# Attention and two expert layers on one core: layer two's first expert taken from a row's choice, gate columns spread during routing, expert lists on VectorE

## The chip, the cores and the metric

The kernel runs on one core of a Trainium2 chip. The metric is the device time of one execution in microseconds (us), the median of several runs. Engines are called TensorE (PE in the profile; PEld is its weight load), VectorE (DVE), ScalarE (ACT), GpSimd (POOL) and SyncE (SP, which here only issues DMAs).

## The reference, cut to what matters

```python
# attention: 4 batches, 8 heads, 768 rows, head width 64; 8 global keys and a band of 96
x = attention(q, k, v)                    # 3072 rows x 512
def layer(x, w_gate, w1, w2, bias):       # 8 experts, w1 512x1024, w2 1024x512 each, float32
    logits = x @ w_gate + bias            # bias only in layer two, by each row's modality
    e = argmax(logits, axis=1)
    for expert in range(8):
        rows = (e == expert)
        if rows.any():
            out[rows] = gate[rows] * (relu(x[rows] @ w1[expert]) @ w2[expert])
```

Layer one, then layer two on its output. The counts of rows by expert follow from the inputs. When the reference is computed, layer one's experts 0 to 7 get 455, 416, 361, 397, 367, 410, 395 and 271 rows. Layer two's get 0, 1503, 0, 1556, 13, 0, 0 and 0. The first row that layer one sends to its expert 0 is row 1, and layer two sends that row to its expert 3.

## The kernel before, in words

**Stages.** Attention runs first (`banded_attention`, which is taken for these sizes; `general_attention` is code for other sizes that every engine jumps over). Then `routing(0)`, `mixture(0)`, `routing(1)` and `mixture(1)`.

**Routing.** `find_rows` on VectorE takes each row's best expert, counts the tiles of 128 rows that each expert needs (`t.te`), and gives each expert its first tile (`t.tb`). One-hot matrices `t.ob` and `t.val` are written; TensorE multiplies them (`count_and_rows`) into the table of source rows, from which the first gather index `t.gidx` comes. In layer two a line forces the count of expert 0 to at least one: `t.te[:, 0, 0:1]` is maximised with 1.0. Expert 0's weights are loaded before layer two's routing is known, and its first tile is always tile 0. `list_experts` on GpSimd makes the list of active experts (`t.e_i`), of their first tiles (`t.tb_i`) and their number (`t.na_i`). All engines wait for it (`s.listed`) before they enter the mixture. `sum_values` on TensorE turns gates and destinations into slots' order; in layer one it stands ahead of the first tile's matmuls, in layer two behind them.

**Mixture.** Tiles of 128 slots are worked on one after another. For tile i TensorE does `up(i)` (24 matmuls, L1080), `turn_x(i+1)` (transposes of the next tile's rows, L1069), `down(i-1)` (24 matmuls, L1100) and `turn_h(i)` (transposes of h, L1088). ScalarE makes h (L1176), the high part of x (L1162) and of h (L1182). VectorE makes the low parts (x: L1198, h: L1246) and the scaled result y (L1226), and in layer one it weighs y with the gate columns `t.wg2` of layer two (L1218), from which layer two's logits come.

**Weights.** An expert's weights are 8 chunks of 512 KB. SP loads them into four stage buffers. In the first tile of an expert, ScalarE copies the eight chunks of the *next* expert into the other half of `t.W` (L1170) and VectorE writes their low parts (L1207, `w_low`). Chunks 1 to 4 stand before the h work of that tile on both engines, chunks 5 to 8 behind it. Chunk 5's load waits until chunk 1's low part is written. In the last expert of layer one, the next expert is layer two's first one. Its first four chunks are issued as soon as the last expert's own weights are split, which is in an earlier expert's tiles.

**Gate columns.** `load_gate2` (SP, L928) broadcasts layer two's gate matrix over 128 partitions into `t.q` and `t.k` once attention is stored. `spread_gate2` (ScalarE, L938) reorders it into `t.wg2`. Since `t.wg2` shares memory with the one-hot tables, it waits for layer one's `sum_values` (`tabled` 2), and stands between the first `x_high` and the first tile's h on ScalarE.

**Attention's end.** `add_logits(B - 1, NPR - 1)` adds the last pair's share of layer one's logits on VectorE (L460). Then VectorE leaves the block, loads the flag `t.banded`, and jumps over the code of `general_attention` to `find_rows` (L758).

Of the kernel before, what the change touches and what calls it, by code (L numbers as in the profile page):

```python
# [30 lines left out]
LISTS = 7  # L31
# [46 lines left out]
def setup_block(nc, t, s, q, k, v, n_global, n_local, w_gate, w_gate2, mod_bias):  # L78

    with nc.Block() as block:  # L80
# [15 lines left out]
        def _(pool):  # L96
            pool.memset(t.ones[:, :], 1.0).then_inc(s.consts, 1)
            pool.memset(t.ident[:, :], 0.0).then_inc(s.consts, 1)
            pool.memset(t.v[:, :, :, DH:VW], 1.0).then_inc(s.consts, 1)
# [12 lines left out]
            pool.wait_ge(s.consts, 2)  # L112
# [44 lines left out]
def banded_attention(t, s, q, k, v, x1, x2, w1, w2, modality_id):  # L157
# [219 lines left out]
    def vector(dve):  # L377
        flag = dve.value_load(t.banded[0:1, 0:1], min_val=0, max_val=1)
        with dve.If_eq(dve.to_reg(flag), 1):
# [117 lines left out]
            add_logits(B - 1, NPR - 1)  # L497
            dve.wait_ge(s.logits_moved, NPR * B + 1)
# [48 lines left out]
    return gpsimd, sync, tensor, vector, scalar  # L547
# [178 lines left out]
def routing(t, s, layer):  # L726
# [6 lines left out]
    st = s.route[layer]  # L733
    L = t.logits[:, 0:nt, :] if layer == 0 else t.logits2[:, 2:2 + nt, :]
# [7 lines left out]
    group = lambda g: t.val[:, 0:nt, g, :]  # L742
    within, total = t.PS[:, 0, 0:nt * E], t.PS[:, 1, 1:1 + nt * E]
    before = t.PS[:, 1, 0:nt * E]

# [10 lines left out]
    def find_rows(dve):  # L756
# [42 lines left out]
        if layer:  # L799
            link(dve, dve.tensor_tensor(col(3), col(3), t.far[:, :], ALU.add))  # L800
# [3 lines left out]
        dve.wait_ge(st.slot_known, 1)  # L804
        place = t.iota_row[:, 0:E + 1].unsqueeze(2).to_broadcast([P, E + 1, E])
# [6 lines left out]
        for i0, i1 in pieces:  # L812
            dve.tensor_tensor(t.ob[:, i0:i1, :], t.iota_row[:, :].unsqueeze(1).to_broadcast([P, i1 - i0, P]),  # L813
                              t.c[:, 2, i0:i1].unsqueeze(2).to_broadcast([P, i1 - i0, P]), ALU.is_equal)\
               .then_inc(st.placed, 1)
# [46 lines left out]
    def list_experts(pool):  # L862
        count = [LISTS * layer]

        def then(ins):

            count[0] += 1
            ins.then_inc(s.listed, 1)
            pool.wait_ge(s.listed, count[0])

        order = t.act[:, 1, :]
        pool.wait_ge(st.ordered, 2)
        a = t.lists[:, :, :, :]
        then(pool.tensor_copy(t.na_i[:, layer:layer + 1], order[:, E:E + 1]))
        then(pool.tensor_tensor(a, a, t.te[:, :, :].unsqueeze(2).to_broadcast([P, 2, E + 1, E]), ALU.mult))

        for w in (4, 2, 1):
            then(pool.tensor_tensor(a[:, :, :, 0:w], a[:, :, :, 0:w], a[:, :, :, w:2 * w], ALU.add))  # L878
        then(pool.tensor_copy(t.tb_i[:, :], a[:, 0, :, 0:1].rearrange("p a e -> p (a e)")))
        then(pool.tensor_copy(t.e_i[:, :], a[:, 1, :, 0:1].rearrange("p a e -> p (a e)")))  # L880

    def exps_and_rows(act):
# [9 lines left out]
        act.activation(t.ob[:, 0:by_act, :], t.apart[:, 0:by_act, :], ACT.Relu, bias=t.ones_f[:, 0:1], scale=-1.0)\  # L892
           .then_inc(st.placed_act, 1)

    def count_and_rows(pe):
        pe.wait_ge(st.chosen, 1)
# [4 lines left out]
        for n, (i0, i1) in enumerate(pieces + [(0, by_act)]):  # L901
            if n < 2:
                pe.wait_ge(st.placed, 2 + n)
            else:
                pe.wait_ge(st.placed_act, 1)
            for i in range(i0, i1):
                last = pe.matmul(t.PS[:, 2, 0:2 * MAXT], t.ob[:, i, :], t.val[:, i, 0:2, :]
                                 .rearrange("p g a -> p (g a)"), start=i == pieces[0][0], stop=i == by_act - 1)
# [680 lines left out]
```

## Time and profile before

| | us |
|---|---|
| median of 3 runs | 1084.35 |
| lowest and highest | 1084.23 and 1086.38 |
| the profiled execution | 1084.99 |
| its span | 1083.3 |
| TensorE matmul busy in it | 977.4 |
| VectorE busy | 619.4 |
| ScalarE busy | 406.5 |
| GpSimd busy | 184.3 |

Start times in the rows below are microseconds from the span's start. A row of the timeline merges neighbours of one kind (x4 is four instructions). Its bracket says how long the engine had been idle before the row and what released it.

### The profile page before, as it was taken

To read this page: it belongs to the slowest core of one execution; us is meant where nothing else is said; L and a number is where in the kernel's file an instruction comes from. 1 tells how busy PE (TensorE), PEld (TensorE's weight loads), DVE (VectorE), ACT (ScalarE), POOL (GpSimd) and SP (SyncE) were. 2 spreads that over 40 slices of the span, in tenths; PEclk is the share of its full clock that TensorE was granted. 3 is DMA by queue.
4 is the path that set the end of the run, shared out by engine and by line. 5 is a ranking of instruction groups with operands and counts; after the bars stand their busy time and mean duration, and the time that the engine had idled before them with its cause. 6 is when DMAs were issued, how large, how long until landed. Compare 5 with 4: busy or idle time off the path is not lost.

```text
span 1083.3 us, 19099 instructions
## 1 busy us (share of the span) xinstructions
PE 977.4 (90%) x5416; PEld 828.4 (76%) x5417; DVE 619.4 (57%) x1584; ACT 406.5 (38%) x735; POOL 184.3 (17%) x275
## 2 busy tenths in 40 slices
PE   4999999999248999999999999356999999999995
PEld 3999999998246888888888888245888888888884
DVE  6666666665439697896987969837322225222221
ACT  3655555553244333343352533206322225222220
POOL 1291000000041111111111111032212112121111
PEclk9999999999569999999999999768999999999998
DMA  9996566401235152451551513026411113111110
GB/s 164 241 266 142 109 133 140 101 27 31 94 107 191 43 194 81 161 194 48 194 180 62 194 48 107 19 98 226 142 39 44 43 39 123 39 39 48 39 39 12
DMA packets 140343, 114.86 MB, mean 106 GB/s; under 512 B 102111, under 2 KB 114447, under 8 KB 140176
## 3 DMA queue, kind: packets, MB, share of 16 engines
q1 hardware_dynamic: 129104, 78.70, 26.4%
q0 software_dynamic: 11200, 35.69, 9.9%
q8 instruction: 19, 0.31, 0.1%
q14 instruction: 20, 0.16, 0.0%
HBM read 91.82 MB, written 23.59 MB: 107 GB/s over the span
## 4 chain that ended last, share of the span: by engine, by line
PE 86%; DVE 4%; issue 4%; POOL 1%; ACT 1%; DMA 1%; SPq 1%; DVEq 1%; ACTq 0%; POOLq 0%
PE PS L1100 28%; PE PS L1080 27%; PE PS L323 7%; PE PS L301 7%; PE PS L1088 4%; PE PS L311 3%; PE PS L1069 2%; PE PS L266 2%; PE PS L287 2%; PE PS L278 1%; ACT gate_columns L938 1%; DVE W L1207 1%; POOL lists L878 1%; DVE ob L813 0%; DMA stage<-in_moe_w_dram 0%
## 5 line engine op out<-in xcount | busy, mean ns | idle before, releaser
L1080 PE MATMUL PS<-W,xT_high 128*128 (+1 forms) x896 | 286.7, 401 | 11.1 <-DVE W L1207 8.6
L1100 PE MATMUL PS<-W,hT_high 128*128 (+1 forms) x896 | 286.5, 401 | 6.8 <-DVE hT_low L1246 6.8
L1080 PEld LDWEIGHTS PS<-W,xT_high 128*128 128x128 f32 x896 | 167.2, 192 | 44.8 <-issue 10.9
L1100 PEld LDWEIGHTS PS<-W,hT_high 128*128 128x128 f32 x896 | 164.2, 188 | 42.9 <-issue 4.4
L1080 PE MATMUL PS<-W,xT_low 128*128 (+1 forms) x448 | 177.2, 395 | 0.0
L1100 PE MATMUL PS<-W,hT_low 128*128 (+1 forms) x448 | 177.0, 395 | 0.0
L1218 DVE CUSTOM_DVE_ANT_0 products<-y,gate_columns 128x512 f32<-128x512 f32 x236 | 148.7, 688 | 0.0
L1182 ACT ACTIVATE hT_high<-PS 128x512 fp32r<-128x512 f32 x112 | 60.9, 597 | 218.9 <-PE PS L1088 218.9
L1176 ACT ACTIVATE h<-PS 128x512 f32<-128x512 f32 x112 | 65.6, 595 | 195.9 <-PE PS L1080 192.6
L1198 DVE TENSOR_TENSOR xT_low<-PS,xT_high 128x512 fp32r<-128x512 f32 x58 | 40.1, 691 | 171.8 <-ACT xT_high L1162 168.5
L538 ACT ACTIVATE pbuf<-biased_scores,nmax 128x256 f32<-128x256 f32 (+1 forms) x192 | 87.3, 488 | 107.2 <-DVE nmax L423 105.8
L1226 DVE TENSOR_SCALAR y<-PS,gate 128x512 f32<-128x512 f32 x58 | 43.5, 750 | 132.4 <-PE PS L1100 131.8
L1170 ACT ACTIVATE W<-stage 128x1024 f32 x88 | 89.6, 1060 | 46.6 <-DMA stage<-in_moe_w_dram 46.6
L1207 DVE TENSOR_TENSOR W<-stage,W 128x1024 f32 x88 | 102.7, 1222 | 6.0 <-ACT W L1170 4.0
L1080 PEld LDWEIGHTS PS<-W,xT_low 128*128 128x128 f32 x448 | 85.5, 191 | 18.7
L1100 PEld LDWEIGHTS PS<-W,hT_low 128*128 128x128 f32 x448 | 84.2, 188 | 20.3
L301 PE MATMUL PS<-kT,qT 128*128 128x256 f32 (+1 forms) x384 | 96.7, 374 | 1.3 <-DVE nmax L423 0.6
L423 DVE CUSTOM_DVE_ANT_0 biased_scores<-PS,bias 128x256 f32<-128x256 f32 (+1 forms) x192 | 72.9, 399 | 22.6 <-issue 11.2
L1007 POOL DMA_INDIRECT xin<-attended,gather_rows x30 | 34.8, 1160 | 240.5 <-issue 216.4
L1246 DVE TENSOR_TENSOR hT_low<-PS,hT_high 128x512 fp32r<-128x512 f32 x112 | 72.0, 685 | 4.4
L323 PE MATMUL PS<-v_rows,pT 128*128 128x65 f32 x384 | 68.5, 274 | 2.1 <-DVE pT L432 2.0
L301 PEld LDWEIGHTS PS<-kT,qT 128*128 128x128 f32 x384 | 61.9, 195 | 5.9 <-DVE nmax L423 1.5
(194 smaller groups left out, 1070.2 us busy)
## 6 DMA issues: line engine op xcount, KB each, us to landing
stage<-in_moe_w_dram SPq DMA_DIRECT2D x88, 512.0 KB, 5.0
mixed<-y POOLq DMA_DIRECT2D x30, 256.0 KB, 2.3
q_rows<-in_q_dram SPq DMA_DIRECT2D x32, 192.0 KB, 3.4
k_rows<-in_k_dram SPq DMA_DIRECT2D x32, 192.0 KB, 3.6
v_rows<-in_v_dram SPq DMA_DIRECT2D x32, 192.0 KB
attended<-x_rows SPq DMA_DIRECT2D x16, 384.0 KB, 3.3
v_before<-in_v_dram SPq DMA_DIRECT2D x32, 150.0 KB
stage<-in_moe_w_dram POOLq DMA_DIRECT2D x8, 512.0 KB, 8.6
```

Of the source, the lines that this page charges most:

```text
L301: last = pe.matmul(t.ps_s[:, n % 3, c:c + w], lhs, t.kT[:, p % 2, k0:k0 + w], start=True, stop=True)
L323: last = pe.matmul(out, lhs, rhs, start=n == 0, stop=n == len(terms) - 1)
L423: dve.tensor_tensor_reduce(out=t.sb[:, n % 3, 0:w], in0=t.ps_s[:, n % 3, c:c + w], in1=t.bias[:, h, o:o + w], scale=-SCALE, scalar=3.0e38, ...
L538: act.activation(t.pbuf[:, h % 2, i, c:c + w], t.sb[:, n % 3, 0:w], ACT.Exp, bias=t.nmax[:, h % 2, i:i + 1], scale=-1.0).then_inc(s.exped, 1)
L1080: last = pe.matmul(t.PS[:, f, :], lhs[:, c, :], t.W[:, bass.ds(w + part, 512)], start=c == 0 and n == 0, stop=c == KD - 1 and n == 2)
L1100: last = pe.matmul(t.PS[:, 2, :], lhs[:, c, :], t.W[:, bass.ds(off + (c * D + part), D)], start=c == 0 and n == 0, stop=c == KF - 1 and n ...
L1170: act.activation(t.W[:, bass.ds(other + k * WCH, WCH)], t.stage[:, k % RING, :], ACT.Copy).then_inc(m.w_hi, 1)
L1176: act.activation(t.h[:, f * 512:(f + 1) * 512], t.PS[:, f, :], ACT.Relu).then_inc(st.h_ready, 1)
L1182: act.activation(t.hTh[:, 4 * f:4 * f + 4, :].rearrange("p c n -> p (c n)"), t.PS[:, 3 + f, :], ACT.Copy).then_inc(st.h_high, 1)
L1207: dve.tensor_tensor(t.W[:, bass.ds(other + (k * WCH + WBUF), WCH)], t.stage[:, k % RING, :], t.W[:, bass.ds(other + k * WCH, WCH)].bitcast ...
L1218: dve.tensor_tensor_reduce(out=t.products[:, e % 2, :], in0=t.y[:, :], in1=t.wg2[:, e, :], scale=1.0, scalar=0.0, op0=ALU.mult, op1=ALU.ad ...
L1246: dve.tensor_tensor(t.hTl[:, 4 * f:4 * f + 4, :].rearrange("p c n -> p (c n)"), t.PS[:, 3 + f, :], t.hTh[:, 4 * f:4 * f + 4, :].rearrange( ...
```

## The change

- The last logits are added in a function of their own, `last_logits`, which stands behind `general_attention`'s code and loads the flag again.
- The expert lists are made on VectorE behind the first gather index, with five instructions instead of seven on GpSimd; `list_experts` is gone.
- `count_and_rows` multiplies ScalarE's part of the one-hot tables first instead of last.
- Layer one's one-hot tables have their own memory (`ob_first`, `val_first`), and `spread_gate2` stands at the end of ScalarE's routing work, without the wait for `tabled`.
- Layer two's first expert is the one that row 0 of tile 0 chose. `first_choice` on VectorE finds it in the first tile of layer one's last expert, behind `x_low`. SP waits for it, reads its number and then issues the load of layer two's first weights.
- Layer two's routing gives tile 0 to that expert and moves the experts ahead of it back; its count is at least 1, and no other count is raised.

```diff
@@ find_rows @@
-        link(dve, dve.tensor_scalar(t.te[:, 0, 0:1], t.te[:, 0, 0:1], 1.0, None, ALU.max))
+        if layer == 0:
+            link(dve, dve.tensor_scalar(t.te[:, 0, 0:1], t.te[:, 0, 0:1], 1.0, None, ALU.max))
+        else:
+            link(dve, dve.tensor_tensor(t.te[:, 0, :], t.te[:, 0, :], star, ALU.max))
+            do(dve, dve.tensor_tensor(t.mine[:, 1:E + 1], t.te[:, 0, :], star, ALU.mult))
...
+        if layer:
+            link(dve, dve.reduce_sum(t.mine[:, 0:1], t.mine[:, 1:E + 1], AX.X))
+            link(dve, dve.scalar_tensor_tensor(t.tb[:, 0:E], ahead, t.mine[:, 0:1], t.tb[:, 0:E],
+                                               ALU.mult, ALU.add))
+            link(dve, dve.scalar_tensor_tensor(t.tb[:, 0:E], star, 0.0, t.tb[:, 0:E], ALU.is_equal, ALU.mult))
...
         if layer:
+            do(dve, dve.tensor_tensor(t.act[:, 1, 0:E], t.act[:, 1, 0:E], ahead, ALU.add))
...
+        if layer:
+            link(dve, dve.scalar_tensor_tensor(t.act[:, 1, 0:E], star, 0.0, t.act[:, 1, 0:E],
+                                               ALU.is_equal, ALU.mult))
...
         dve.tensor_copy(t.gidx[:, :], t.src[:, 0:1]).then_inc(st.src_ready, 1)
+        dve.wait_ge(st.ordered, 2)
+        link(dve, dve.tensor_tensor(t.lists[:, :, :, :], t.lists[:, :, :, :],
+                                    t.te[:, :, :].unsqueeze(2).to_broadcast([P, 2, E + 1, E]), ALU.mult))
+        link(dve, dve.tensor_reduce(t.list_f[:, :], t.lists[:, :, :, :].rearrange("p l a e -> p (l a) e"),
+                                    axis=AX.X, op=ALU.add))
+        dve.tensor_copy(t.tb_i[:, :], t.list_f[:, 0:E + 1]).then_inc(s.listed, 1)
+        dve.tensor_copy(t.e_i[:, :], t.list_f[:, E + 1:2 * E + 2]).then_inc(s.listed, 1)
+        dve.tensor_copy(t.na_i[:, layer:layer + 1], t.act[:, 1, E:E + 1]).then_inc(s.listed, 1)
@@ count_and_rows @@
-        for n, (i0, i1) in enumerate(pieces + [(0, by_act)]):
-            if n < 2:
-                pe.wait_ge(st.placed, 2 + n)
+        for n, (i0, i1) in enumerate([(0, by_act)] + pieces):
+            if n:
+                pe.wait_ge(st.placed, 1 + n)
@@ spread_gate2 @@
     act.wait_ge(s.wg2_loaded, 32)
-    act.wait_ge(s.route[0].tabled, 2)
@@ mixture, sync @@
-            load(next_w1, next_w2, 0, after.w_loaded,
+            sp.wait_ge(s.star_known, 3)
+            e = sp.value_load(t.star_i[0:1, 0:1], min_val=0, max_val=E - 1)
+            load(next_w1, next_w2, e, after.w_loaded,
@@ mixture, vector @@
+        def first_choice():
+            now = t.logits2[:, 2, :]
+            best, rank, picked = t.star_f[:, 0:1], t.star_f[:, 1:2], t.star_f[:, 3:3 + E]
+            dve.reduce_max(best, now, AX.X).then_inc(s.star_chain, 1)
...
         def tile(i, j, other, m):
             x_low(i + 1)
+            if m is not None and m is not st:
+                first_choice()
@@ stages @@
             banded_dve(dve)
             general_dve(dve)
+            last_logits(dve)
             find0(dve)
...
             exps0(act)
+            spread_gate2(act, t, s)
             act.wait_ge(s.listed, LISTS)
```

VectorE between attention and routing, before: the add of the logits, then the way over the general code. The first fence is the end of attention's block; the second is where the jump arrives.

```order
L723 TENSOR_SCALAR cols_b<-modf 128x24 [waits modality_chain]
L460 TENSOR_TENSOR logits<-logits,PS 128x48 [waits logits_moved,logits_read]
L379 UNCONDITIONAL_BRANCH [waits logits_moved]
L641 TENSOR_LOAD banded
L641 ISA x2
L642 COMPARE_AND_BRANCH
```

```order
L758 MEMSET PS 128x1
L759 MEMSET tb 128x1
```

The same two places of VectorE in the changed kernel, first the end of attention's block, then where the jump arrives.

```order
L733 TENSOR_SCALAR cols_b<-modf 128x24 [waits modality_chain]
L381 UNCONDITIONAL_BRANCH
L651 TENSOR_LOAD banded
L651 ISA x2
L652 COMPARE_AND_BRANCH
```

```order
L548 TENSOR_LOAD banded
L548 ISA x2
L549 COMPARE_AND_BRANCH
L553 TENSOR_TENSOR logits<-logits,PS 128x48 [waits logits_moved,logits_read]
L549 UNCONDITIONAL_BRANCH [waits logits_moved]
L770 MEMSET PS 128x1
L771 MEMSET tb 128x1
```

The add, with its wait for TensorE, has moved from in front of the long jump to behind it, and a second short load and branch stand around it.

VectorE in the changed kernel, in the first tile of layer one's last expert, from the subtraction for the next tile's x to the first weighing of y: seven small instructions are new.

```order
L1214 TENSOR_TENSOR xT_low<-PS,xT_high 128x512
L1257 TENSOR_REDUCE star_f<-logits 128x1
L1259 SCALAR_TENSOR_TENSOR star_f<-logits,star_f,rank_e 128x8
L1262 TENSOR_REDUCE star_f<-star_f 128x1
L1264 TENSOR_SCALAR star_f<-star_f 128x1
L1266 TENSOR_SCALAR star_i<-star_f 128x1
L1267 TENSOR_SCALAR star<-rank_e,star_f,p 128x8
L1269 TENSOR_SCALAR star<-rank_e,star_f,p 128x8
L1231 REGISTER_ALU
```

And SP behind them, at the head of the load of layer two's first weights.

```order
L1016 TENSOR_LOAD star_i [waits star_known]
L1016 ISA x2
L1018 REGISTER_ALU
L1004 ISA [waits w_lo_0]
L1004 DMA stage<-in_moe_w_dram 128x1024
```

SP used to come to these DMAs with a wait for `w_lo_0` alone; now it waits for VectorE's choice first.

## Rows read from the trace of the kernel before

**Rows 1.** The page's slices: busy tenths of TensorE in 40 slices of the span.

```profile
PE   4999999999248999999999999356999999999995
```

**Rows 2.** Timeline of VectorE, layer two, line 1226: first and last of 25 rows.

```profile
767.52 0.75 DVE L1226 TENSOR_SCALAR y<-PS,gate 128x512 f32<-128x512 f32 x1 [2.79 <-PE PS L1100]
...
1065.01 0.75 DVE L1226 TENSOR_SCALAR y<-PS,gate 128x512 f32<-128x512 f32 x1 [4.43 <-PE PS L1100]
```

**Rows 3.** Timeline of ScalarE, layer two, line 1170: chunks 1 to 4 of a set.

```profile
731.67 3.88 ACT L1170 ACTIVATE W<-stage 128x1024 f32 x4
749.87 3.90 ACT L1170 ACTIVATE W<-stage 128x1024 f32 x4
898.60 3.90 ACT L1170 ACTIVATE W<-stage 128x1024 f32 x4
```

**Rows 4.** Timeline of layer two's start, 685 to 769 us.

```profile
712.18 1.26 DVE L837 TENSOR_TENSOR val<-val,cols_b 128x1024 bf16<-128x1024 bf16 x1
719.46 1.22 PE L1080 MATMUL PS<-W,xT_high 128*128 x2 [1.67 <-DVE xT_low L1198]
735.17 0.69 DVE L1198 TENSOR_TENSOR xT_low<-PS,xT_high 128x512 fp32r<-128x512 f32 x1 [3.11 <-issue]
740.58 1.06 ACT L1170 ACTIVATE W<-stage 128x1024 f32 x1 [4.06 <-DMA stage<-in_moe_w_dram]
740.60 1.21 PE L1080 MATMUL PS<-W,xT_high 128*128 x2 [8.59 <-DVE W L1207]
755.54 0.71 PE L1080 MATMUL PS<-W,xT_high 128*128 x2
```

**Rows 5.** Windows: length; PE, PEld, DVE, ACT, POOL busy us; PEclk, DMA share, GB/s.

```profile
741.00:746.00 5.00, 5.00 (x13) 3.83 (x13) 4.06 (x6) 3.17 (x4) 2.03 (x2) 0.50 0.95 322
```

**Rows 6.** Timeline of layer one's start, 288 to 342 us.

```profile
302.15 3.12 DVE L837 TENSOR_TENSOR val<-val,gate 128x768 bf16<-128x768 bf16 x3
305.99 0.19 POOL L880 CAST e_i<-lists 128x9 int32<-128x9 f32 x1
309.06 3.41 PE L914 MATMUL PS<-val,ob 128*128 128x160 bf16 x24
318.61 2.04 ACT L938 ACTIVATE gate_columns<-k_rows 128x1024 f32<-128x1024 f32 x1
323.35 1.97 PE L1088 MATMUL PS<-ident,h 128*128 128x128 f32 x8 [4.84 <-ACT h L1176]
325.06 1.22 PE L1080 MATMUL PS<-W,xT_high 128*128 128x512 f32 x2
```

**Rows 7.** Timeline of VectorE between attention and routing.

```profile
273.88 0.18 DVE L723 TENSOR_SCALAR cols_b<-modf 128x24 bf16<-128x24 f32 x1
278.48 0.20 DVE L460 TENSOR_TENSOR logits<-logits,PS 128x48 f32<-128x48 f32 x1 [4.42 <-PE PS L287]
286.00 0.06 DVE L758 MEMSET PS<- 128x1 f32 x1 [7.31 <-issue]
```

**Rows 8.** DMA view: window 284 to 285 us by queue; window 277 to 278 by issue.

```profile
q14 instruction: 1, 0.01, 1.9%
...
q_rows<-in_moe_w_gate_dram SPq DMA_DIRECT2D x1, 1536.0 KB, 7.6
```

**Rows 9.** Timeline of the first tile of layer one's last expert.

```profile
646.41 0.69 DVE L1198 TENSOR_TENSOR xT_low<-PS,xT_high 128x512 fp32r<-128x512 f32 x1 [2.65 <-ACT xT_high L1162]
655.23 1.28 DVE L1246 TENSOR_TENSOR hT_low<-PS,hT_high 128x512 fp32r<-128x512 f32 x2
657.85 0.72 PE L1100 MATMUL PS<-W,hT_high 128*128 x2
663.41 0.69 DVE L1198 TENSOR_TENSOR xT_low<-PS,xT_high 128x512 fp32r<-128x512 f32 x1
```

**Rows 10.** SP's issues from 307.86 us; GB/s in 40 slices of 307 to 317 us.

```profile
307.86 34.14 SPq L988 DMA_DIRECT2D stage<-in_moe_w_dram  x12
...
GB/s 0 0 0 0 0 0 0 180 66 279 377 393 360 393 443 459 377 328 328 164 180 147 262 279 262 377 344 442 410 393 426 393 442 213 246 180 131 115 49 0
```

More of the change, by code:

```diff
@@ L30 @@
 WBUF = NCH * WCH
-LISTS = 7
+LISTS = 3
 RING = 4
@@ L545, in scalar, with last_logits @@
             run_slots(act, slot)
-    return gpsimd, sync, tensor, vector, scalar
+    def last_logits(dve):
+        flag = dve.value_load(t.banded[0:1, 0:1], min_val=0, max_val=1)
+        with dve.If_eq(dve.to_reg(flag), 1):
+            now = t.logits[:, (B - 1) * NQ:B * NQ, :]
+            dve.wait_ge(s.logits_read, NPR * B)
+            dve.wait_ge(s.logits_moved, NPR * B)
+            dve.tensor_tensor(now, now, t.ps_lg[:, 0:NQ * E].rearrange("p (i e) -> p i e", e=E), ALU.add)\
+               .then_inc(s.logits_moved, 1)
+            dve.wait_ge(s.logits_moved, NPR * B + 1)
+    return gpsimd, sync, tensor, vector, last_logits, scalar
 def general_attention(t, s, q, k, v, x1):
@@ L733, in routing @@
     st = s.route[layer]
+    ob, val = t.ob[layer], t.val[layer]
     L = t.logits[:, 0:nt, :] if layer == 0 else t.logits2[:, 2:2 + nt, :]
@@ L741, in routing @@
     slots = lambda a: a.unsqueeze(2).to_broadcast([P, nt, MAXT])
-    group = lambda g: t.val[:, 0:nt, g, :]
+    group = lambda g: val[:, 0:nt, g, :]
     within, total = t.PS[:, 0, 0:nt * E], t.PS[:, 1, 1:1 + nt * E]
     before = t.PS[:, 1, 0:nt * E]
+    star, ahead = t.PS[:, 2, 2 * MAXT:2 * MAXT + E], t.PS[:, 2, 2 * MAXT + E:2 * MAXT + 2 * E]
     def do(dve, ins):
@@ L860, in take_values @@
             dve.sem_inc(s.tab_ready, 1)
[L862 to L880, printed above, removed]
     def exps_and_rows(act):
@@ L891, in exps_and_rows @@
         act.wait_ge(st.apart, by_act)
-        act.activation(t.ob[:, 0:by_act, :], t.apart[:, 0:by_act, :], ACT.Relu, bias=t.ones_f[:, 0:1], scale=-1.0)\
+        act.activation(ob[:, 0:by_act, :], t.apart[:, 0:by_act, :], ACT.Relu, bias=t.ones_f[:, 0:1], scale=-1.0)\
            .then_inc(st.placed_act, 1)
     def count_and_rows(pe):
+        if layer:
+            pe.wait_ge(s.star_known, 3)
+            pe.matmul(t.PS[:, 2, 2 * MAXT:2 * MAXT + 2 * E], t.ones[:, :],
+                      t.star[:, :, :].rearrange("p a e -> p (a e)"), start=True, stop=True)
         pe.wait_ge(st.chosen, 1)
@@ L906, in count_and_rows @@
             for i in range(i0, i1):
-                last = pe.matmul(t.PS[:, 2, 0:2 * MAXT], t.ob[:, i, :], t.val[:, i, 0:2, :]
-                                 .rearrange("p g a -> p (g a)"), start=i == pieces[0][0], stop=i == by_act - 1)
+                last = pe.matmul(t.PS[:, 2, 0:2 * MAXT], ob[:, i, :], val[:, i, 0:2, :]
+                                 .rearrange("p g a -> p (g a)"), start=i == 0, stop=i == nt - 1)
         last.then_inc(st.tabled, 1)
@@ L913, in sum_values @@
         for i in range(nt):
-            last = pe.matmul(t.PS[:, 7, 0:(groups - 2) * MAXT], t.ob[:, i, :],
-                             t.val[:, i, 2:groups, :].rearrange("p g a -> p (g a)"), start=i == 0, stop=i == nt - 1)
+            last = pe.matmul(t.PS[:, 7, 0:(groups - 2) * MAXT], ob[:, i, :],
+                             val[:, i, 2:groups, :].rearrange("p g a -> p (g a)"), start=i == 0, stop=i == nt - 1)
         last.then_inc(st.tabled, 1)
-    return find_rows, take_values, list_experts, exps_and_rows, count_and_rows, sum_values
+    return find_rows, take_values, exps_and_rows, count_and_rows, sum_values
 DQ = NQ * D // E
@@ L1031, in gpsimd @@
         fetch(0)
-        list_experts(pool)
+        pool.wait_ge(s.listed, LISTS * (layer + 1))
         tiles = pool.value_load(t.tb_i[0:1, E:E + 1], min_val=E, max_val=MAXT - 1)
@@ L1186, in scalar @@
         x_high(0)
-        if layer == 0:
-            spread_gate2(act, t, s)
         experts(act, tile)
@@ L1421, in program @@
             t.lg_now = sb("lg_now", [P, E], F32, a)
+        with ExitStack() as o:
+            sb("beside_first_and_rows", [P, 2 * WBUF + 2 * NQ * D], F32, o)
+            ob0 = sb("ob_first", [P, NT, P], BF16, o)
+            val0 = sb("val_first", [P, NT, 8, MAXT], BF16, o)
         t.W = sb("W", [P, 4 * WBUF], F32R)
```

48 lines of the change are left out of this document (35 added, 13 removed).

## The prediction

> **What bounds the kernel now.** I read the page's slices first, then the timeline at each place where they dip. TensorE is busy in nine tenths or more of nearly every slice but for two dips, at slices 11 to 13 and 26 to 28 [rows 1]: the ways from attention into layer one and from layer one into layer two. In between it is the bound. In layer two the scaled result is written once a tile; 25 such rows lie between 767.52 and 1065.01, so a tile costs 297.49 / 24 = 12.40 us whatever the other engines do [rows 2]. A change can then gain in three ways only: fewer tiles, shorter dips, or a wait less inside the chain of tiles. It can lose by a new wait in that chain.
>
> The reader should see one thing more. In the first tile of each expert ScalarE splits the weights of the next. In layer two those sets start at 731.67, 749.87 and 898.60 [rows 3]. The first is tile 0, the second starts 18.2 us later, and the third 148.7 us after that, 12 x 12.4. So the first expert has one tile, and the second twelve. The counts by expert in the reference say that expert 0 has no row at all in layer two. This tile is forced and empty.
>
> **Part 1: layer two's first expert is one with rows.** Row 0 of tile 0 is a row that goes to expert 3, which has 1556 rows, 13 tiles. The raised count then raises nothing, so there are 26 tiles (13, 12 and 1) and no longer 27. One tile less: **12.4 us** [rows 2].
>
> **Part 2: layer two's start.** Before, tile 1 belonged to another expert, whose weights were still to be split: its first matmul came at 740.60 after 8.59 us of waiting for a low part [rows 4], and TensorE then ran at the lower of its two levels, half the clock, until about 746 [rows 5]. Tile 2 began at 755.54 [rows 4]. Now tiles 0 to 12 have one expert, and tile 1 needs only x. I go step by step.
> - Routing. Seven small VectorE instructions are new and one is replaced. A short instruction with its own wait costs about 0.2 us and one that needs none 0.08 (starts of neighbours in this routing): five and two make some 1.06 us. ScalarE's part first in the multiplication takes about half of the last stretch of small matmuls off, 0.6. The lists cost VectorE 1.2 (a product and a sum of 144 elements at 0.3 each with their waits, and three casts). The last value table, done at 712.18 + 1.26 = 713.44 [rows 4], is then done at 715.1. The memset (0.5) and the low part of x (0.7) follow, since the lists are there long before, and the first matmul comes at 716.6 instead of 719.46 [rows 4]: 2.85 earlier.
> - Tile 1's low part of x comes behind the reading of registers on VectorE, at 735.17 before [rows 4], now at 732.3; the first matmul of tile 1 is at 733.1 instead of 740.60.
> - Its 24 matmuls take 5.6 at the full clock. Then VectorE and ScalarE bind: the second group of weight chunks waits for loads, the first of these until 740.58 before [rows 4], now 2.8 earlier. The four copies end at 743.9 instead of 746.7, h takes 2.4 more, the parts of x for tile 2 another 1.2, and tile 2 begins at 747.5 instead of 755.54.
>
> So **8.0 us**, of which 2.85 come from routing. From below: if TensorE falls to the lower level in its wait of some 4 us before tile 1, half of tile 1's matmuls take twice as long, but ScalarE's chain mostly covers that; 6 remain. From above 9.5, if h did not have to wait for the copies.
>
> **Part 3: layer one's start.** GpSimd's list ended at 305.99 + 0.19, and the value tables on VectorE at 302.15 + 3.12 = 305.27 [rows 6]. The list is now ready near 300.4, and is no longer last. The gathered rows are, near 304. The value tables now end at 305.27 + 1.2 - 0.5 (lists, and the earlier table) = 305.9. The 24 small matmuls behind them take 3.4 [rows 6], so `up(0)` starts near 309.2 and ends at 314.8. Before, its h waited for the gate columns on ScalarE, which ended at 318.61 + 2.04 and were followed by 2 us of register reads; TensorE idled 4.84 us for it [rows 6]. Now these 8.2 us stand at the end of ScalarE's routing (296.6 to 304.9), where ScalarE had nothing to do. Without that cover they would cost 8.2. h follows at once, the parts of x for tile 1 end at 316.9, and tile 1's first matmul comes at 316.9 instead of 325.06 [rows 6]: **8.15 us**. What follows (weights, y, low part of h) has the same order and moves along. Bounds 6 and 9.
>
> **Part 4: the last logits and the long jump.** The add ran at 278.48, and routing began at 286.00: 7.31 us in which VectorE waited for nothing but its own instructions [rows 7]. The way over the general code has one load and one far branch. Now VectorE starts it at 273.88 + 0.18, beside TensorE's last logits, and the add behind it. If the way costs the same 7.3, it arrives at 281.4. With one more short load and near branch (about 1 us) and the add, routing starts at 282.9: 3.1 us gained. If the way costs less, up to 7.2 can be gained (the add can't come ahead of TensorE's 278.45). There is a sign that it will: an instruction packet of queue 14 is moved between 284 and 285, in the midst of the broadcast of 1536 KB that takes 7.6 us to land, and VectorE goes on 1.5 us later [rows 8]. The new jump is made before that broadcast is issued. I take **5.5 us**, bounds 3 and 7.
>
> The Trainium skill (Runtime: NRT & Kernel Launch, Instruction fetch mechanics) says that a taken branch to a target outside the fetched window has to fetch it by DMA before execution goes on; the trace agrees, with the packet ahead of 286.00. The Trainium skill (DMA: Bandwidth & Descriptors, Queues, rings and completion order) has each DMA engine take turns between queues, switching only after a whole packet of descriptors. If turns were short, the fetch would hardly wait for the broadcast, the way would cost its 7.3 us anywhere, and the sum would be 2.4 us smaller; no row here shows how long a turn was.
>
> **Part 5: the new wait.** SP used to issue the first four chunks for layer two tiles ahead. Now it waits for the choice in the first tile of the last expert. `x_low` ends there at 646.41 + 0.69 = 647.1 [rows 9]; the seven instructions take 1.16, the register read 0.9, so the first chunk is issued at 649.2. How long a group of four takes shows at 307.86: data flows from 309 to 317, the first chunk there after some 3.4 us, and the others every 1.6 [rows 10]. They land at 652.6, 654.2, 655.8 and 657.4. ScalarE copies each in 1.06 and VectorE subtracts in 1.2, so the fourth low part is done near 659.7, and behind it wait y, the low parts of h (655.23 before, near 660.5 now), the weighing and chunks 5 to 8. TensorE needs h's low part at 657.85, and has 1.3 us of slack [rows 9]. It loses 4 there. Chunks 5 to 8 follow without gaps, and the low part of x behind them, at 663.41 before [rows 9], comes at 668.8. Its slack is 0.2, so the loss grows to **-5.3 us**. Bounds -4 and -7. It isn't given back, since TensorE is the bound behind it.
>
> **Sum.** 12.4 + 8.0 + 8.15 + 5.5 - 5.3 = 28.75. From the profiled execution's 1084.99 this gives 1056.2, and from the median of 1084.35 it gives 1055.6 us.
>
> **The rivals.**
> - *The four chunks share the queue and land together.* For it: they are issued within 2 us and the rows show only the sum of their traffic. Against: before, chunks that ScalarE waited for came one by one. Then chunk 1 is there at 657.4, not 652.6, and the same again for chunks 5 to 8 in part. The loss is about 10 and the time 1060.
> - *The tile stays.* The change would not do what it says if the chosen expert had no tile of its own, or the order of the lists still began with expert 0. Then part 1 and most of part 2 (but for routing's 2.85) are gone: 17.5 us less, 1073. Against it stand the counts: a row that exists chooses, and its expert has 13 tiles.
> - *Slower: the clock after the new wait.* TensorE idles some 5 us in part 5. After 8.59 us of idling it ran half as fast for 5.3 us [rows 4, 5]. If it stayed at the lower level for the three tiles of layer one's last expert and on, each would cost some 11 us more. It decides from 29 us on, that is from three such tiles: 1087. Against it: it came back within one tile, and in layer one it idled 4.84 without a stretch of slow matmuls [rows 6].
> - *Better than the sum.* VectorE arrives before TensorE's last logits and h is never late: 7.2 in part 4 and 9.5 in part 2: 1052.
>
> **How the numbers follow.** The forecast, with its bounds, has 0.75; landing together 0.10; the tile stays 0.03; slower 0.02; better than 1052 0.10. The range takes the forecast's bounds together as far as they are likely (part 4 at 3, part 5 at -7, part 2 at 6 would give 1062): 1051 to 1061, which also holds the case of chunks that land together. A measurement can tell about 0.2%, 2.2 us, from no change. Only the clock ends on the other side, and no case gives a sum near zero: faster 0.97, same 0.01, slower 0.02.
>
> **What would show it.** Layer two has 27 rows of the scaled result and not 28, two sets of weight copies and not three, and tile 1's first matmul comes without an 8.6 us wait. In layer one the transposes of h don't wait for ScalarE. VectorE's add stands behind the jump and routing starts within 0.5 us of it. SP's wait for the choice is seen as a gap before the last set's copies on ScalarE, and one of some 4 to 5 us on TensorE. The prediction is wrong if the fetch meets the broadcast again (a later page of code), or if the wait for the choice costs more than 7.

## The result and the profile after

| | before | changed |
|---|---|---|
| median | 1084.29 | 1060.32 |
| lowest and highest of 4 runs | 1083.08 and 1086.38 | 1059.44 and 1061.21 |
| the profiled execution, its span | 1084.99, 1083.3 | 1059.44, 1057.6 |

The ratio is 0.9777, 95% interval [0.976, 0.9794]: 24.0 us faster, where 28.75 were predicted. Timed once more, on the chip of the first experiments, it is 1059.74 and 0.9774.

TensorE's slices on the page of the changed kernel:

```profile
PE   4999999999478999999999998628999999999995
```

The first dip is shallower than in [rows 1] (4, 7 and 8 where 2, 4 and 8 stood). The second has changed its shape more than its size: 8, 6, 2 and 8 lack twelve tenths of busy time, where 3, 5 and 6 lacked thirteen. None is gone. The reader should now go to the places of the sum, one by one.

**Attention's end.** Timeline of VectorE, against [rows 7]:

```profile
274.95 0.18 DVE L733 TENSOR_SCALAR cols_b<-modf 128x24 bf16<-128x24 f32 x1
279.79 0.20 DVE L553 TENSOR_TENSOR logits<-logits,PS 128x48 f32<-128x48 f32 x1 [4.66 <-PE PS L289]
280.27 0.06 DVE L770 MEMSET PS<- 128x1 f32 x1 [0.28 <-DVE logits L553]
```

Attention ended 1.07 later in this execution (it does so from 273.9 to 276.6 in the fourteen traces of this study). Routing started 5.73 earlier, so 6.8 were gained. The bracket names TensorE, but the chain that ended last shows what the 4.66 us were. Its columns are start, length and what the time went to (a q marks the engine's sequencer, which loads registers and branches):

```profile
275.13 0.15 DVEq L651
...
275.68 3.31 issue
278.98 0.32 DVEq L548
279.33 0.19 DVEq L548
279.79 0.22 DVE logits L553
```

L651 is the flag's load ahead of the long branch, L548 the one behind it. The branch itself took 3.31 ("issue" is time in which the engine waited for nothing that the profile shows). Before, flag, branch and arrival took 7.31 together, behind TensorE's last logits; now most of them run beside those.

**Layer one's start.** Timelines of ScalarE and TensorE, against [rows 6]:

```profile
296.46 2.03 ACT L954 ACTIVATE gate_columns<-k_rows 128x1024 f32<-128x1024 f32 x1
...
310.65 0.74 PE L1098 MATMUL PS<-W,xT_high 128*128 128x512 f32 x2 [0.56 <-DVE xT_low L1214]
```

The columns are spread long before h, and the transposes of h wait for nothing. Tile 1 came 14.41 earlier than 325.06, of which 5.73 are routing's: 8.7.

**The last switch.** VectorE, SP, ScalarE and TensorE in the first tile of layer one's last expert, then VectorE and TensorE at the tile behind it, against [rows 9]:

```profile
632.79 0.69 DVE L1214 TENSOR_TENSOR xT_low<-PS,xT_high 128x512 fp32r<-128x512 f32 x1 [2.67 <-ACT xT_high L1180]
635.61 1.91 SPq L1004 DMA_DIRECT2D stage<-in_moe_w_dram  x4
639.48 2.27 ACT L1188 ACTIVATE W<-stage 128x1024 f32 x2 [6.73 <-DMA stage<-in_moe_w_dram]
643.80 1.06 ACT L1188 ACTIVATE W<-stage 128x1024 f32 x1 [0.18 <-DMA stage<-in_moe_w_dram]
648.36 1.21 PE L1118 MATMUL PS<-W,hT_high 128*128 x2 [3.89 <-DVE hT_low L1283]
...
655.03 0.68 DVE L1214 TENSOR_TENSOR xT_low<-PS,xT_high 128x512 fp32r<-128x512 f32 x1
657.62 0.70 PE L1098 MATMUL PS<-W,xT_high 128*128 x2
```

The last row's place in the kernel before:

```profile
664.33 0.71 PE L1080 MATMUL PS<-W,xT_high 128*128 x2
```

The issue stands 2.8 behind `x_low`, the first chunk is copied 3.9 later and the fourth 8.2 later. TensorE idled 3.89 us. Then the clock fell. In windows of the same stretch the last three numbers are TensorE's granted clock, the DMA engines' busy share and GB/s:

```profile
644.00:648.00 4.00, 0.47 (x5) 0.23 (x3) 3.98 (x5) 3.01 (x5) 0.31 (x1) 0.96 0.83 283
648.00:652.00 4.00, 3.64 (x9) 2.87 (x10) 4.00 (x11) 2.98 (x4) 1.98 (x3) 0.50 0.73 279
652.00:656.00 4.00, 4.00 (x14) 3.14 (x13) 4.00 (x5) 1.42 (x3) 0.00 (x0) 0.69 0.16 50
```

The changed kernel led by 13.6 at this tile's `x_low` (646.41 against 632.79), and by 6.7 at the next tile's first matmul (664.33 against 657.62) and at layer one's last scaled result: 6.9 lost. The next low part of x stands 22.2 behind this one (22.4 by the prediction's working), and TensorE came to its next tile 1.9 after it was done, without a bracket: by then it was its own slower matmuls that it had to finish.

**Layer two's start and its tiles.** TensorE and VectorE, against [rows 2, 4]:

```profile
709.56 1.22 PE L1098 MATMUL PS<-W,xT_high 128*128 x2 [3.84 <-DVE xT_low L1214]
724.58 1.22 PE L1098 MATMUL PS<-W,xT_high 128*128 x2 [3.93 <-DVE xT_low L1214]
...
751.32 0.75 DVE L1242 TENSOR_SCALAR y<-PS,gate 128x512 f32<-128x512 f32 x1 [4.42 <-PE PS L1118]
1036.44 0.75 DVE L1242 TENSOR_SCALAR y<-PS,gate 128x512 f32<-128x512 f32 x1 [4.44 <-PE PS L1118]
```

751.32 answers to 767.52, 16.2 earlier, of which 6.7 came with it: 9.5 gained. A part of that is the clock in tile 0. The first five us behind its first matmul, before and changed:

```profile
719.46:724.46 5.00, 5.00 (x12) 3.94 (x13) 0.00 (x0) 0.00 (x0) 0.46 (x1) 0.50 0.84 282
709.56:714.56 5.00, 5.00 (x16) 4.02 (x17) 0.00 (x0) 0.58 (x1) 0.00 (x0) 0.71 0.87 285
```

From the first matmul of tile 0 to that of its last took 8.20 before and 6.74 here. In the second profile of the changed kernel it took 8.24, and layer two's start gained 8.7 and not 9.5.

1036.44 answers to 1065.01, 28.57 earlier: one tile of 12.4 more. Layer two has 27 scaled results.

**The end.** TensorE's last down matmuls, GpSimd's last scatter, and the window of the matmuls (granted clock 0.66):

```profile
1039.05 0.73 PE L1118 MATMUL PS<-W,hT_high 128*128 x2 [1.98 <-DVE hT_low L1283]
1050.21 1.00 POOL L1044 DMA_INDIRECT out_dram<-y,scatter_rows  x1 [2.35 <-issue]
```

```profile
1039.00:1044.00 5.00, 4.95 (x15) 3.92 (x16) 0.00 (x0) 0.00 (x0) 0.55 (x1) 0.66 0.10 39
```

The last scaled result came 10.25 behind the one ahead of it, against 8.70 before, and the last scatter waited 2.35 where it had waited 0.88. So 2.9 were lost that no term of the prediction held.

Sum of the pair: 12.4 + 9.5 + 8.7 + 6.8 - 6.9 - 2.9 - 1.1 (attention) - 0.8 (two intervals between scaled results of layer one that were 0.35 longer, and rounding) = 25.7, the difference of the spans.

### The profile page after: what moved, and what is told of

It is laid out like the page before. It is cut to its first block, busy times and chain, and to the rows that moved or that the text cites. A ratio compares the mean times of both kernels' runs of the same rounds, so it can differ in the third digit from the quotient of the medians.

```text
span 1057.6 us, 18804 instructions
## 1 busy us (share of the span) xinstructions
PE 968.1 (92%) x5357; PEld 819.4 (77%) x5358; DVE 611.5 (58%) x1595; ACT 395.6 (37%) x722; POOL 173.4 (16%) x259
## 3 DMA queue, kind: packets, MB, share of 16 engines
q1 hardware_dynamic: 127440, 74.51, 26.4%
## 4 chain that ended last, share of the span: by engine, by line
PE 85%; DVE 6%; issue 3%; DMA 2%; ACT 1%; SPq 1%; DVEq 1%; POOL 0%; ACTq 0%; POOLq 0%
PE PS L1118 28%; PE PS L1098 27%; PE PS L325 8%; PE PS L303 7%; PE PS L1106 4%; PE PS L313 4%; PE PS L268 2%; PE PS L1087 2%; PE PS L289 2%; DMA stage<-in_moe_w_dram 1%; PE PS L280 1%; DVE val L870 1%; DVE W L1223 0%; ACT W L1188 0%; DMA k_rows<-in_k_dram 0%
## 5 line engine op out<-in xcount | busy, mean ns | idle before, releaser
L1098 PE MATMUL PS<-W,xT_high 128*128 (+1 forms) x880 | 279.6, 399 | 8.4 <-DVE xT_low L1214 8.3
L1098 PEld LDWEIGHTS PS<-W,xT_high 128*128 128x128 f32 x880 | 163.1, 190 | 41.0 <-DVE xT_low L1214 5.3
L1098 PE MATMUL PS<-W,xT_low 128*128 (+1 forms) x440 | 173.5, 394 | 0.0
L1188 ACT ACTIVATE W<-stage 128x1024 f32 x80 | 81.8, 1059 | 52.0 <-DMA stage<-in_moe_w_dram 51.5
L1223 DVE TENSOR_TENSOR W<-stage,W 128x1024 f32 x80 | 93.5, 1221 | 8.5 <-ACT W L1188 6.4
(224 smaller groups left out, 1057.6 us busy)
```

The lines of the kernel that those rows point to most:

```text
L1098: last = pe.matmul(t.PS[:, f, :], lhs[:, c, :], t.W[:, bass.ds(w + part, 512)], start=c == 0 and n == 0, stop=c == KD - 1 and n == 2)
L1188: act.activation(t.W[:, bass.ds(other + k * WCH, WCH)], t.stage[:, k % RING, :], ACT.Copy).then_inc(m.w_hi, 1)
L1223: dve.tensor_tensor(t.W[:, bass.ds(other + (k * WCH + WBUF), WCH)], t.stage[:, k % RING, :], t.W[:, bass.ds(other + k * WCH, WCH)].bitcast ...
```

## The experiments

All times are medians in us, and ratios are to the kernel before on the same chip. The changed kernel again, expert 0 first, the add in front and the columns late were timed against a before of 1084.63; the lists, the late broadcast, the choice in the last expert but one and the additional load against 1084.89; the other four against 1083.75.

**The changed kernel again.**

> The changed kernel itself, as the measure for the others of this call. Every theory: 1060 us against 1084 for the kernel before. In its profile the gap of 3.9 us before the down matmuls of the first tile of layer one's last expert and the low clock behind it should be there again, and TensorE's idling of about 2 us before the last tile's down as well. If the last tile's down runs at the full clock this time, the 1.5 us that it cost belong to one execution.

Measured: 1059.74. TensorE idled 4.31 at the last switch and the clock fell behind it, and again at the end. Neither belongs to one execution. The faster tile 0 of layer two was not there this time.

**Expert 0 first again.**

```diff
-            sp.wait_ge(s.star_known, 3)
-            e = sp.value_load(t.star_i[0:1, 0:1], min_val=0, max_val=E - 1)
-            load(next_w1, next_w2, e, after.w_loaded,
+            load(next_w1, next_w2, 0, after.w_loaded,
...
-            if m is not None and m is not st:
-                first_choice()
```

> The changed kernel with expert 0 as layer two's first expert again: no choice, no wait of SP for it, count of expert 0 forced to one. My theory, by terms: the empty tile returns (+12.4), layer two's start loses what the one expert gained without routing (+6.5), and the wait in layer one's last expert is gone (-6.9): +12.0, so 1072.3 us. The rival, that the wait costs only the 5.3 that I predicted and the low clock behind it belongs to one execution: +13.6, 1073.9. In the profile TensorE should not idle before down in layer one's last expert, and layer two should have 28 rows of the scaled result.

Measured: 1068.35, so the choice of the expert, all in all, is worth 8.6 us. Both numbers on record were too high. The terms come from its profile against that of the changed kernel in the same call, whose span is 8.6 shorter: the tile 12.4; layer two's start 3.0 and not 6.5, since without the choice routing is 1.1 shorter (26.4 from its start to the first matmul, against 27.5), since 1.5 of the 6.5 don't hang on the choice, and since some 0.8 of them was the clock in the first profile; the wait -5.7, for here the clock fell at layer one's last down instead; the end -2.9, which I had left out. With 1.7 that attention and layer one's start took more in this execution, that is 8.5, and the spans' 8.6 but for rounding.

**The add in front of the jump.**

```diff
             modality(t, s, dve)
+            add_logits(B - 1, NPR - 1)
+            dve.wait_ge(s.logits_moved, NPR * B + 1)
...
-            last_logits(dve)
```

> The changed kernel with the last logits added in front of the long jump again. My theory (the far code is fetched beside the broadcast of the gate matrix, and that makes the way 7.3 us long): routing starts 6.5 to 7 us later, 1066.8 us. The rival (the way costs the same 7.3 us wherever the add stands, and only TensorE's last logits were hidden): +3.1, 1063.4. In both an instruction packet is seen after the broadcast is issued.

Measured: 1066.39, +6.65. The rival's 3.1 is excluded. VectorE:

```profile
279.42 0.20 DVE L462 TENSOR_TENSOR logits<-logits,PS 128x48 f32<-128x48 f32 x1 [4.43 <-PE PS L289]
286.63 0.06 DVE L772 MEMSET PS<- 128x1 f32 x1 [7.01 <-issue]
```

**Before, with the broadcast late.** This is the same question asked of the kernel before.

```diff
     sp.wait_ge(s.attended, 1)
+    sp.wait_ge(s.route[0].chosen, 1)
     for dst, d0, d1 in ((t.q, 0, DQ), (t.k, DQ, D)):
```

> The kernel before, with one more wait: SP issues the broadcast of layer two's gate matrix only when VectorE has finished finding the rows' experts in layer one's routing, so behind the long jump. My theory (the fetch of the far code waits for the broadcast's packets): the jump takes 3 to 4 us less, layer one's routing starts at 282 instead of 286.0, and the total is 3.5 to 4.5 less, 1080.3 us; the gate columns are spread behind it without being late, since they waited for the value tables anyway. The rival (the way over the general code costs 7.3 us whatever the queues do): routing starts at 286.0 as before, 1084.3 us.

Measured: 1082.08, ratio 0.9974 [0.9963, 0.9985]: 2.8 us, interval 1.6 to 4.0; its profiled span is 2.9 shorter. Against [rows 7]:

```profile
278.70 0.20 DVE L460 TENSOR_TENSOR logits<-logits,PS 128x48 f32<-128x48 f32 x1 [4.42 <-PE PS L287]
282.68 0.06 DVE L758 MEMSET PS<- 128x1 f32 x1 [3.78 <-issue]
```

The same instructions on the same way take 3.78 us instead of 7.31, with nothing moved but the broadcast. In narrow windows of the DMA view, queue 14's instruction packet at the jump stands at 280.7, against 284.1 before; the packet ahead of it stands at 278.5 and 278.3. The fetch waited for the broadcast. The Trainium skill (DMA: Bandwidth & Descriptors, Queues, rings and completion order) says that an engine switches queues only after a whole packet of descriptors; that fits a wait of 3.5 us behind a broadcast that takes 7.6 to land, but no row shows the turns themselves.

**The gate columns late.**

```diff
             exps0(act)
-            spread_gate2(act, t, s)
...
+    act.wait_ge(s.route[0].tabled, 2)
...
         x_high(0)
+        if layer == 0:
+            spread_gate2(act, t, s)
```

> The changed kernel with the gate columns spread behind layer one's first high part of x again, waiting for the value tables. My theory: the 8.2 us on ScalarE stand between x and h of tile 0 again, h waits, and TensorE idles some 5 us before the transposes of h: +5 to +6, 1065.8 us. The rival: the gain of 8.7 us at layer one's start is all the spreading's, then +8.7, 1069. A second rival: with the list made earlier the spreading ends before h is ready, then nothing, 1060.3.

Measured: 1063.96, +4.2; from routing's start to the first scaled result it is 42.95 against 37.90 and 37.63 in the two profiles of the changed kernel, so +5.1 in the trace. TensorE waits for h as in [rows 6]:

```profile
314.69 1.92 PE L1107 MATMUL PS<-ident,h 128*128 128x128 f32 x8 [4.51 <-ACT h L1195]
```

**The lists on GpSimd.** VectorE's five instructions are gone and GpSimd's seven stand between its first gather and the mixture again.

```diff
-        dve.tensor_copy(t.tb_i[:, :], t.list_f[:, 0:E + 1]).then_inc(s.listed, 1)
...
-        pool.wait_ge(s.listed, LISTS * (layer + 1))
+        list_experts(pool)
```

> The changed kernel with the expert lists made by seven instructions on GpSimd again. My theory: in layer one GpSimd's list is last again, about 5 us behind VectorE's, and TensorE's value tables and the first tile come that much later; in layer two it is off the path. +4 to +5 in all, 1064.8 us. The rival: the value tables on VectorE (1.2 us shorter without the lists) are what binds in both layers, then -1 to +1, 1060.

Measured: 1067.49, +7.75 (6.7 by the two ratios), more than either number. Layer one's start is 4.5 longer as I said, but the list binds in layer two too, which I had denied. GpSimd and TensorE in layer two's routing:

```profile
707.28 3.54 POOL L903 TENSOR_TENSOR lists<-lists 128x72 f32<-128x72 f32 x3
711.15 0.20 POOL L905 CAST e_i<-lists 128x9 int32<-128x9 f32 x1
...
714.12 1.11 PE L1099 MATMUL PS<-ident,xin 128*128 128x128 f32 x4 [11.58 <-issue]
```

TensorE's row comes 2.8 us behind the list, and the first matmul stands 31.1 behind routing's start, against 27.5. Its idle time is put down to "issue", that is to register reads and branches, which come behind the wait for the list. In the kernel before, the list ended at 714.04 and the same matmuls stood at 716.68. Three small GpSimd operations take 3.54 us here and 1.56 in layer one, where VectorE's multiplications beside them are three quarters as wide. That the two engines slow each other was not tested.

**The choice in the last expert but one.** The choice is made in that expert's first tile on VectorE, so that SP never waits.

```diff
+            one(eng.snap((n + 6) % 8), early)
...
         one(eng.snap(n - 1), after)
...
-            if m is not None and m is not st:
+            if m == "choose":
                 first_choice()
+                m = st
```

> The changed kernel with the choice of layer two's first expert made in the first tile of the last expert but one, so that SP's wait for it is long over when the last expert's own weights are split. It assumes that layer one has at least two active experts and that tile 0's logits are there by then. My theory: TensorE's wait of 3.9 us before down and the low clock behind it go, 6.9 us in all, 1053.4 us. The rival: the load of layer two's first chunks is late for another reason (it is issued behind the last expert's split anyway), then 5.3 or less is had, 1055 or more.

Measured: 1056.21, -3.5 (4.3 by the two ratios). The wait is gone: the intervals between scaled results at the last switch are 15.46, 12.38 and 9.35 us, where the changed kernel has 20.66, 12.38 and 11.04. But the tile with the choice and the next take 16.82 and 13.11 instead of 15.5 and 12.4. The seven instructions cost 2.0 there, ahead of the low parts of weights and the loads that those release. The clock also fell at layer one's last down, 1.5.

**The choice between two experts.** It is made on VectorE ahead of a low part of x that VectorE waits 2.7 us for.

```diff
+            with eng.If(n > 2):
+                with eng.Fori(0, n - 2) as j:
+                    one(j, st)
+            early()
+            one(eng.snap((n + 6) % 8), st)
...
-            if m is not None and m is not st:
-                first_choice()
```

> The changed kernel with the choice made on VectorE between layer one's last expert but two and last but one, so ahead of a low part of x for which VectorE waits 2.7 us anyway (it assumes two active experts at least, and tile 0's logits by then). In the kernel with the choice in the last expert but one's first tile, TensorE's wait in the last expert was gone, but the seven instructions stood ahead of four weighings, a low part of weights and chunk 5's load, and that tile and the next lost 1.3 and 0.7. My theory: here these 2.0 are had too, 1054.2 us against 1056.2, and the intervals between the scaled results are 15.5, 12.4, 9.3 as in the experts ahead. The rival: the 2.0 come from another cause (the code is longer), then 1056.2 again.

Measured: 1053.76, ratio 0.9726 [0.9713, 0.9739], the fastest kernel of the study: 5.2 us below the changed kernel by the two ratios. The intervals are 15.53, 12.38, 9.28 and 12.38 at the expert with the choice and 15.47, 12.38, 9.35 and 8.66 at the last: the seven instructions cost nothing. VectorE still waits 1.38 behind them for the high part of x. It holds only where layer one has two active experts at least and the row's logits are there two experts ahead of the end; the changed kernel waits for the last expert and needs neither.

**TensorE kept busy in the wait.**

```diff
             turn_x(i + 1)
+            if last is not None:
+                with pe.If(last < 1):
+                    for e in range(4):
+                        pe.matmul(t.PS[:, 7, :], t.ident[:, :], t.wg2[:, e, :], start=True, stop=True)
```

> The changed kernel with four float32 matmuls of 512 columns between TensorE's transposes of x and its down matmuls, in the first tile of layer one's last expert alone; their result is read by nobody. They fill some 3.4 of the 3.9 to 4.3 us in which TensorE waits for the low part of h there. My theory: the fall of the clock behind this wait comes of the idling, so the down matmuls run at the full clock, and 1.7 us of the tail of layer one are had: 1058.2 us. They may be lost again at layer one's last down, where in other kernels the clock fell after 1.9 us of idling; then the sum of the last four intervals between the scaled results stays at 53 us and the total at 1059.7. The rival: the clock falls whatever TensorE does there, and the total is 1059.7 or, with the four matmuls past the wait, more.

Measured: 1058.75, ratio 0.9765 [0.9752, 0.9778], which can't be told from 0.9774. The matmuls ran at 632.1 already, ahead of the down of the tile before, and pushed the work behind them back by 3.2 us, so the idle time is gone all the same. TensorE at down, and the window behind it:

```profile
648.78 0.73 PE L1118 MATMUL PS<-W,hT_high 128*128 x2 [0.69 <-DVE hT_low L1287]
```

```profile
648.00:652.00 4.00, 3.31 (x15) 2.66 (x15) 4.00 (x10) 2.16 (x3) 2.29 (x3) 1.00 0.78 284
```

The clock stays at full speed, and the next interval is 9.22 instead of 11.04. What is left of the wait is 20.91 + 12.38 + 9.22 against 37.14 before, 5.4 us: the size of the predicted term. But then the clock fell at layer one's last down, as the expectation allowed:

```profile
670.80 0.73 PE L1118 MATMUL PS<-W,hT_high 128*128 x2 [1.97 <-DVE hT_low L1287]
```

```profile
672.00:676.00 4.00, 4.00 (x13) 3.09 (x12) 3.42 (x13) 0.00 (x0) 0.00 (x0) 0.57 0.00 0
```

**One more load by GpSimd.** At the start GpSimd loads the modality ids a second time, into a tensor that nothing reads.

```diff
+        pool.dma_start(t.modi2[:, :, :], modality_id.bitcast(I32)
+                       .rearrange("(i p w) -> p i w", p=P, w=2)).then_inc(s.modality_loaded, 16)
```

> The changed kernel with one more load by GpSimd at the start, of the same modality ids into a tensor that nothing reads. My theory: the gap of 2.35 us before the last scatter comes after a fixed number of GpSimd's DMAs, so it moves to the scatter before the last one, where it is hidden: -1.5, 1058.8 us, and the last scatter waits 0.9 us or so. The rival: the gap belongs to the last scatter or to the one execution, or one more DMA at the start doesn't count: 1060.3 us, and the gap stands where it stood.

Measured: 1061.2, ratio 0.9787 [0.977, 0.9803], no gain. The last scatter still waits 2.35. The theory falls as put: it isn't the count of all of GpSimd's DMAs.

**One more indirect gather.**

```diff
+        if layer == 0:
+            pool.indirect_dma_start(out=t.extra_rows[:, :], out_offset=None, in_=src[:, :],
+                                    in_offset=bass.IndirectOffsetOnAxis(ap=t.gidx[:, 0:1], axis=0))\
+                .then_inc(s.extra_loaded, 16)
+            pool.wait_ge(s.extra_loaded, 16)
```

> The changed kernel with one more indirect gather by GpSimd in layer one, into a tensor that nothing reads. In four kernels the wait of 2.35 to 2.39 us stands before the 84th indirect DMA of the program, which is the last scatter with 26 tiles in layer two and the last but two with 27; a direct load more didn't move it. My theory: it goes with the count of indirect DMAs, so now it stands before the last but one and is hidden; the last scatter waits 0.9, -1.4 us, 1058.4. The rival: it comes with something else at that place, and stays before the last scatter: 1059.8.

Measured: 1062.76, ratio 0.9814 [0.98, 0.9827], 3 to 4 us slower than the changed kernel. Half of the theory held: the last scatter no longer waits. But it did not move, as the theory says, to the 84th indirect DMA, which is the last but one here and waits 1.11.

```profile
1038.73 1.01 POOL L1044 DMA_INDIRECT out_dram<-y,scatter_rows  x1 [1.11 <-issue]
1048.70 1.00 POOL L1044 DMA_INDIRECT out_dram<-y,scatter_rows  x1 [0.89 <-POOL scatter_rows L1041]
```

But the span ends 11.9 us behind the last scatter's start (1060.6), where it is 7.4 in the changed kernel (1057.6 - 1050.21) and 7.4 to 7.6 in every other without the gather. The data land 2.3 us after the issue as ever. The 4.5 us more stand in GpSimd's closing drain, of the changed kernel and of this one:

```profile
L1327 POOLq DRAIN  x1: 4811/4811/4811, 1052.6 to 1052.6; - x1
L1332 POOLq DRAIN  x1: 9302/9302/9302, 1051.1 to 1051.1; - x1
```

The first three numbers are its duration in ns. Behind it stand only the closing semaphores, and it takes 4.8 to 5.0 us in every kernel without the gather. What it waits for stays open.

**Both.**

> The choice between the experts and the additional indirect gather, both. If both theories hold, the gains add up: 5.5 and 1.4 off 1059.7, 1052.8 us. If only the first holds, 1054.2; if only the second, 1054.8 or more.

Measured: 1058.02, ratio 0.9758 [0.9744, 0.9771]: 4.3 slower than with the choice between the experts alone. From the last scatter to the end it is 11.9 again, with a drain of 9.30, so the loss comes with the added gather. It is no gain.

## Why the prediction was right, and where it was off

The time lies in the range, 4.7 us above the forecast of 1055.6. 1.5 of that is which executions were profiled: that of the changed kernel was 0.9 below its median, that of the kernel before 0.6 above the median on record. The other 3.1 or so are between the sum of 28.75 and the 25.7 of the pair: one loss was taken too small (1.6), others had no term (the end 2.9, attention 1.1, the two intervals 0.8), and three gains were larger than said (3.3 together). That the number stayed inside the range is so in part luck: had the gains come out as worked, it would have been near 1063.6.

**Part 1, one tile less, 12.4:** 12.4, as read.

**Part 2, layer two's start, 8.0:** 9.5. The routing's share was right, 27.5 us against 30.5, so 3.0 for 2.85. The seven new instructions cost what was said: without the choice it is 1.1 less. The last stretch of small matmuls took 0.77 for 1.30, also as said, though the new order of the multiplication was not tested by itself. In the changed kernel VectorE's value tables do bind, and the lists are there 7.8 us before them, as on record. What the working left out is that in the kernel before the tables, done at 713.44, were not the last to arrive: GpSimd's list came at 714.04. The gain therefore hangs on moving the list, which is worth 3.6 us in layer two. The rest gained 6.5, not 5.15, and the difference is the clock: tile 0's matmuls took 1.5 less because the lower level ended sooner, and in the second profile tile 1 began 16.5 behind tile 0, just as worked. TensorE did fall to the lower level in its wait before tile 1 (3.93 us; 0.50 from 724.5 to 728), and this cost nothing that the working had not covered.

**Part 3, layer one's start, 8.15:** 8.7, step by step as put. Taken back alone, the columns cost 5.1 in the trace and the lists 4.5. That is more than 8.7 together: with both in place, each hides a part of the other.

**Part 4, the jump, 5.5:** 6.8, within the bounds. Of the two readings that it weighed, the second held: with the fetch beside the broadcast the way takes 7.0 to 7.3, away from it 3.8, shown from both sides.

**Part 5, the new wait, -5.3:** -6.9, and this is the mis-sized term. The delays of x_low, choice, register read and chunks came out as worked, and the idle time was 3.89 for 4. What was missing is the clock. The rival on record let the clock fall for three tiles or not at all; it fell within one tile, and cost some 1.7 us. What it had against a fall was misread: in [rows 6] the eight transposes behind the idle 4.84 take 1.97 us, where eight such take 1.03 at the full clock, and the granted clock there is 0.50 from 323 to 326. So the kernel before already held a short fall behind an idle time of this length. With TensorE busy in the wait the term is 5.4, and with the choice made where VectorE idles it is nothing. The record named a wait of more than 7 as a sign of being wrong; 6.9 is just below it.

**No term:** the end, -2.9. The last down matmuls ran at the lower level (-1.5), and the last scatter met a wait that had stood before the last but two (-1.4). The second comes with part 1 itself: with a tile less the 84th indirect DMA is the last. Why a wait stands there is not shown.

Chunks that land together are excluded by the copies, which begin 3.9 us behind the first issue and not 8.2, where the fourth stands. That rival's 1060 is close to the measured time by chance alone. The tile did not stay: there are 27 scaled results, and 80 copies of weight chunks for 88.

## What to carry to other kernels

A wait that is added for a piece of data is best removed by asking where else the data are known already and which engine idles there: in one trace each, the same seven instructions cost 7, 2 and 0 us at three places (by the ratios of the times, the second place is 4.3 us and the third 5.2 us better than the first). It pays to look whether a far branch stands beside a large transfer, and to move one of them: in the kernel before, delaying the transfer was worth 2.8 us (1.6 to 4.0). When the number of tiles changes, look at what stands behind the last one, since a stall that was hidden in the middle can become the end.

## What the runs showed of the hardware

- The same far branch on VectorE took 3.8 us, and 7.0 to 7.3 when a broadcast of 1536 KB had been issued just before.
- TensorE's granted clock falls to the lower level behind some idle times of 1.9 to 2.0 us and not behind others at the same place. At layer one's last down it fell in 5 of 14 traces, at layer two's in 9 of 14, for 1.5 us each time. When it was kept from falling at one place (the busy wait) it fell at the next. What decides it stays open.
- The wait of 2.35 to 2.39 us of GpSimd stands before its 84th indirect DMA whatever the tiles are, in the profiles with 84 to 86 of them and no added gather. A direct DMA more doesn't move it. With a gather added ahead the 84th and 85th wait 1.11 and 0.89, and GpSimd's closing drain takes 9.30 us instead of 4.81, in both kernels that had it.
